# Outputs of a pair and scores of the next in one visit of TensorE, with another plan of steps and another order at the seam

## The reference

```python
batch, n_heads, seq, head_dim = (4, 8, 768, 48)      # d_model 384
for t in range(S):                                     # per batch b and head h
    state = alpha[:, :, t, :, None] * state + einsum('bhd,bhe->bhde', k[:, :, t], v[:, :, t])
    y[:, :, t] = einsum('bhd,bhde->bhe', q[:, :, t], state)
x = y.transpose(0, 2, 1, 3).reshape(B * S, H * D)      # 3072 tokens x 384
g = relu(x @ moe_w_in) ** 2;  x = g @ moe_w_out        # d_ff 2048
h = x @ moe2_w_in;            out = silu(h) @ moe2_w_out
```

## Time and profile before

| | us |
|---|---|
| median of 3 runs | 881.25 (881.04 to 883.57) |
| the profiled execution, its own time | 879.24 |
| its span | 877.6 |
| PE busy with products | 862.9 (98% of the span) |
| DVE busy | 542.7 (62%) |
| ACT busy | 436.4 (50%) |
| granted clock of PE | full in the whole span |

### The profile page before, as it was taken

How to read it: one execution, slowest core, us unless ns; L and a number is a source line. 1 busy time by engine, 2 the same in 40 slices (tenths; PEclk the granted TensorE clock), 3 DMA queues, 4 the chain that set the end, 5 groups by cost and what they waited for, 6 DMA issues and landing times.

```text
span 877.6 us, 17615 instructions
## 1 busy us (share of the span) xinstructions
PE 862.9 (98%) x6834; PEld 707.4 (81%) x6834; DVE 542.7 (62%) x1072; ACT 436.4 (50%) x770; POOL 104.5 (12%) x127
## 2 busy tenths in 40 slices
PE   6999989999999999999999999999999999999998
PEld 6777768788878788788888788888888888888898
DVE  7788876777767667664344556556855445766620
ACT  5765544455446445544666644445534436554510
POOL 3453300000000000000344003003030003000000
PEclk9999999999999999999999999999999999999999
DMA  8985424333333332300412362000130000110010
GB/s 171 239 227 124 99 66 120 74 75 103 71 82 87 101 79 67 103 19 15 147 49 66 61 116 72 0 1 1 44 102 0 1 1 1 36 37 1 1 48 28
DMA packets 134203, 60.03 MB, mean 68 GB/s; under 512 B 81824, under 2 KB 129312, under 8 KB 134112
## 3 DMA queue, kind: packets, MB, share of 16 engines
q1 hardware_dynamic: 130800, 58.14, 26.9%
q10 hardware_dynamic: 3312, 0.69, 0.4%
HBM read 45.02 MB, written 9.44 MB: 62 GB/s over the span
## 4 chain that ended last, share of the span: by engine, by line
PE 93%; DVE 4%; issue 1%; ACT 1%; DMA 0%; DVEq 0%; ACTq 0%
PE z_ps L1146 21%; PE h_ps L1132 21%; PE h_ps L1175 20%; PE z_ps L1211 11%; PE jobs L1211 7%; PE jobs L1231 3%; PE jobs L1007 1%; PE jobs L1040 1%; PE jobs L1109 1%; DVE decay L1703 1%; PE jobs L1018 1%; PE jobs L1117 1%; PE h_ps L1231 1%; DVE decay L1688 1%; PE z_ps L1078 0%
## 5 line engine op out<-in xcount | busy, mean ns | idle before, releaser
L1429 ACT ACTIVATE g<-h_ps 128x512 f32<-128x512 f32 x96 | 57.4, 597 | 177.6 <-PE h_ps L1132 175.5
L1523 ACT ACTIVATE sum<-sum 128x512 f32<-128x512 f32 x96 | 60.5, 630 | 139.0 <-DVE sum L1871 115.1
L1810 DVE TENSOR_TENSOR g_lo<-g,g_hi 128x512 fp32r<-128x512 f32 x96 | 67.5, 704 | 85.4 <-ACT g L1435 85.4
L1871 DVE TENSOR_TENSOR sum<-h_ps,sum 128x512 f32<-128x512 f32 x120 | 82.8, 691 | 54.2 <-PE h_ps L1175 51.6
L1132 PE MATMUL h_ps<-x_hi,win_hi 128*128 128x512 f32 x288 | 115.0, 399 | 1.2 <-ACT g L1429 0.8
L1146 PE MATMUL z_ps<-g_hi,wout_hi 128*128 128x512 f32 x282 | 114.4, 406 | 0.0
L1132 PE MATMUL h_ps<-x_hi,win_lo 128*128 128x512 f32 x288 | 112.4, 390 | 0.0
L1132 PE MATMUL h_ps<-x_lo,win_hi 128*128 128x512 f32 x288 | 112.2, 389 | 0.0
L1146 PE MATMUL z_ps<-g_hi,wout_lo 128*128 128x512 f32 x282 | 110.2, 391 | 0.0
L1146 PE MATMUL z_ps<-g_lo,wout_hi 128*128 128x512 f32 x282 | 110.1, 390 | 0.0
L1175 PE MATMUL h_ps<-s_hi,t_hi 128*128 128x512 f32 x264 | 103.3, 391 | 0.8 <-DVE sum L1871 0.8
(11 more groups left out here) (169 smaller groups left out, 1544.1 us busy)
## 6 DMA issues: line engine op xcount, KB each, us to landing
z_scratch<-z_sb SPq DMA_DIRECT2D x18, 256.0 KB, 2.6
pre<-z_scratch SPq DMA_DIRECT2D x18, 256.0 KB, 3.8
v_sb<-in_v SPq DMA_DIRECT2D x44, 96.0 KB, 2.6
out_x<-z_stage SPq DMA_DIRECT2D x80, 48.0 KB, 1.7
nat_a<-in_alpha SPq DMA_DIRECT2D x40, 88.0 KB, 2.3
nat_k<-in_k SPq DMA_DIRECT2D x40, 88.0 KB, 2.4
nat_q<-in_q SPq DMA_DIRECT2D x40, 88.0 KB, 2.3
nat_a<-in_alpha SPq DMA_DIRECT2D x40, 80.0 KB, 2.7
```

Source lines behind the costliest of these rows:

```text
L1429: nc.scalar.activation(g[f % 2][:], h_ps[f % 2][:], ACT.Relu).then_inc(act_made, 1)
L1523: nc.scalar.activation(at[:], at[:], ACT.Silu).then_inc(silu_made, 1)
L1810: nc.vector.tensor_tensor(low, g[f % 2][:], high.bitcast(F32), ALU.subtract).then_inc(g_lo_made, 1)
L1871: nc.vector.tensor_tensor(to[:], h_ps[(PRODUCTS * n + r) % 2][:], other[:], ALU.add).then_inc(summed, 1)
```

## The change

Three things change.

1. *One visit.* For pairs n = 8 and later, Y(n) stands in the step of S(n + 1), and ahead of it on PE, so that both are made in one visit between the first and the second product. The output part from the state no longer goes to job_ps[2] but to the bank of h that the step before used (`later_y(n)`), and so S no longer waits for the addition of y. In its place, Y waits for the relu that read that bank and for the addition of the pair before, and the first product of the next step, which writes that bank again, waits for the addition of this y. ACT's copy of y and DVE's addition, which spanned both banks in one instruction, become two each. DVE does the additions right behind the masks of the scores.
2. *Another plan of steps.* Pairs 8 to 11 have their S in steps 16, 18, 21, 24 (before 16, 18, 22, 26), their A in 13, 16, 19, 22 (before 13, 16, 19, 23) and KQ in 14, 17, 20, 23 (before 14, 17, 21, 25). Pairs 12 and later have S in 4 n - 20 in place of 4 n - 18, A in 4 n - 23 in place of 4 n - 21, KQ in 4 n - 21 in place of 4 n - 19. Y(n) stays in 4 n - 16 from pair 11 on.
3. *The seam.* In group 0 ACT copies the last z banks behind the bank of P5 instead of ahead of it; in the first 8 groups DVE adds the bank of P3 ahead of v_lo instead of behind it.

```diff
@@ stage_step
-    if n == 2 * PAIRS:
-        return {"A": 13, "KQ": 14, "S": 16, "I": 16, "Y": 17}[kind]
-    return {"A": -20 if n == 2 * PAIRS + 1 else -21, "KQ": -19, "S": -18, "I": -18, "Y": -16}[kind] + 4 * n
+    if kind == "Y":
+        return stage_step("S", n + 1)
+    if n < 3 * PAIRS:
+        return {"A": (13, 16, 19, 22), "KQ": (14, 17, 20, 23), "S": (16, 18, 21, 24), "I": (16, 18, 21, 24)}[kind][n - 2 * PAIRS]
+    return {"A": -23, "KQ": -21, "S": -20, "I": -20}[kind] + 4 * n
@@ beside
-    return sorted(jobs, key=lambda j: ("S", "I", "A", "Y", "KQ").index(j[0]))
+    return sorted(jobs, key=lambda j: ("Y", "S", "I", "A", "KQ").index(j[0]))
+def beside_scores(n):
+    return n >= 2 * PAIRS
@@ build
-        first_y, middle_y, later_y = z_ps[1], z_ps[0], (job_ps[2], job_ps[0])
+        first_y, middle_y = z_ps[1], z_ps[0]
+        def later_y(n):
+            return (h_ps[(stage_step("Y", n) - 1) % 2][:] if beside_scores(n) else job_ps[2], job_ps[0])
@@ PE, s_stage
-                if n > PAIRS:
+                if n > PAIRS and not beside_scores(n - 1):
                     wait(pe, y_copied, y_count(n))
@@ PE, y_halves
+                if beside_scores(n):
+                    wait(pe, y_copied, y_count(n))
+                    wait(pe, act_made, stage_step("Y", n))
@@ PE, loop over the steps, ahead of first_product
+                for kind, n in beside(F - 1):
+                    if kind == "Y" and beside_scores(n):
+                        pe.wait_ge(y_copied, y_count(n + 1))
@@ ACT, y_copy
+                if beside_scores(n):
+                    to = y_sb[n % 2][:].rearrange("p (c k t) -> p k c t", c=BATCH, k=2)
+                    for k in (0, 1):
+                        last = nc.scalar.activation(to[:, k], later_y(n)[k][0:ROWS, UT // 2:].rearrange("p (c t) -> p c t", c=BATCH),
+                                                    ACT.Copy)
+                    last.then_inc(within_copied, 1)
+                    return
@@ ACT, group n of the second layer
                 tile_step(n, C11)
-                if n == 0:
-                    copy_z(UNITS - 1, UNITS - 1, UNITS - 1)
...
                 spread_second(n)
...
                 if q == 0:
                     for f in v_group(j):
                         v_split(f)
+                if n == 0:
+                    copy_z(UNITS - 1, UNITS - 1, UNITS - 1)
                 tile_step(n, C12)
@@ DVE, y_stage
+                if beside_scores(n):
+                    for k in (0, 1):
+                        to = y_sb[n % 2][:, k * UT // 2:(k + 1) * UT // 2]
+                        last = nc.vector.tensor_tensor(to, later_y(n)[k][0:ROWS, 0:UT // 2], to, ALU.add)
+                    last.then_inc(y_copied, 1)
+                    return
@@ DVE, loop over the steps
                 for kind, n in jobs_here:
                     if kind == "S":
                         s_stage(n)
+                for kind, n in jobs_here:
+                    if kind == "Y" and beside_scores(n):
+                        y_stage(n)
+                for kind, n in jobs_here:
                     if kind == "KQ":
...
-                    if kind == "Y" and n != 2 * PAIRS - 1:
+                    if kind == "Y" and n != 2 * PAIRS - 1 and not beside_scores(n):
                         y_stage(n)
@@ DVE, group n of the second layer
+                dve.wait_ge(summed, PRODUCTS * n + U4_AT)
+                from_bank(n, P3, s_b[2], s_b[2])
                 if q == 0:
                     for f in v_group(j):
                         low_v(f)
-                dve.wait_ge(summed, PRODUCTS * n + U4_AT)
-                from_bank(n, P3, s_b[2], s_b[2])
```

More of the change, by code:

```diff
@@ L1103, in to @@
                     rows = slice(0, 64) if b < 2 else head_rows(1)
-                    return later_y[bank][rows, place * HALF:(place + 1) * HALF], 64 if b < 2 else HD
+                    return later_y(n)[bank][rows, place * HALF:(place + 1) * HALF], 64 if b < 2 else HD
                 for half in (0, 1):
```

## The result

| | before | changed |
|---|---|---|
| median, us | 881.79 (878.98 to 884.40, 22 runs) | 884.46 (881.57 to 889.18, 22 runs) |
| the profiled execution, its own time | 879.24 | 882.96 |
| its span | 877.6 | 881.2 |

The ratio of changed to before is 1.0033, with a 95% interval of 1.0024 to 1.0043: slower by 0.3%.

A forecast was written before the change was run, and what follows sets the result against it. PE, busy 862.9 of 877.6 us, was taken as the bound. Terms -3.4 - 2.5 + 1.5 + 4.5 + 5.4 - 0.9 = +4.6 took 879.24 to 883.8, a median of 886.0 us; range 878.5 to 891.

The forecast's parts named there:

- Visits: On PE, Y(8) to Y(22) join S(9) to S(23): 15 visits fewer at 0.23 us each, -3.4 us.
- Old and new wait of S(9): In step 18, S(9) stops waiting for y's addition, -2.5 us, but waits for q instead, +1.5 us.
- S(10) and S(11): With pairs 10 and 11 three steps apart, both scores wait 2.3 us for q, behind DVE's queue: +4.5 us.
- Rival 1: The new waits do not come, DVE's chain to q being 2.3 us shorter; median 876, chance 0.15.
- Unit edges: At pairs 13, 17, 21 the split of x enters the chain to q: 1.8 us three times, +5.4 us.
- y's addition at no cost: The two y additions end 1.0 us before the next first product starts, so they cost nothing.
- Seam: In the first Strassen group, the new order of copies and additions starts P4 at 502.9 instead of 503.76: -0.9 us.
- rival 4: PE's clock falls to its lower level for one step after each of five new waits: +20 us, median 906, chance 0.02.
- From the profiled execution to the median: The median of timed runs was taken to stand 2.0 us above the profiled execution: 883.8 became 886.0.

The follow-up runs named there:

- e6: e3 with outputs made ahead of the last three of nine large first products and scores behind them, so visits are separate again; 879.98 us, ratio 0.9982 to before.
- e1: The changed kernel with A(10) and A(11) one step earlier (18 and 21); 878.59 us, ratio 0.9956 to the kernel before.
- e2: The changed kernel with A(13), A(17), A(21) one step earlier (28, 44, 60); 879.83 us, ratio 0.9977 to the kernel before.
- e10: e3 with DVE's additions of y about 0.9 us later, ahead of the rest of the I work; 872.34 us, ratio 0.9890 to the kernel before.
- e7: e3 with DVE adding y behind its work for the state instead of right behind the masks; 911.75 us, ratio 1.0336 to the kernel before.
- e4: The kernel before with only the new order at the seam; 880.92 us, ratio 0.9985 to the kernel before.
- e9: e3 with four extra transposes of k on DVE for six pairs, to make their scores wait; 885.40 us, ratio 1.0038 to the kernel before.
- e8: e3 with five extra transposes of k on DVE for six pairs, to make their scores wait; 897.68 us, ratio 1.0187 to the kernel before.
- e3: The changed kernel with A one step earlier for every pair from 10 on; 871.90 us, ratio 0.9889 to the kernel before.
- e5: e3 with S(9) to S(11) in steps 19, 22, 25, pairs 8 to 11 evenly spaced; 871.78 us, ratio 0.9885 to the kernel before.

## Why the prediction was right, and where its terms were off

- **Visits**, forecast -3.4, measured -5.4. The mechanism was right, the size off. The term counted only the 0.23 of a single visit and took the 1.08 of the small work as fixed. In a joined visit the outputs take 0.97, 0.11 less; e6 gave both parts back. This stood within the bounds of 0 to -6.9.
- **Old and new wait of S(9)**, forecast -2.5 and +1.5, measured the same. Here and for S(10) and S(11) two parts were off and cancelled, which is luck: S starts 0.10 after q is ready (122.60 and 122.70), where 0.26 was taken over from the wait for y, and PE comes 0.11 earlier, because Y is shorter.
- **S(10) and S(11)**, forecast +4.5, measured +4.6, and e1 shows the cause: with A ahead of the g_lo that waits for ACT, both are gone. Rival 1 of the prediction named this very difference (in the earlier pairs, three steps apart as well, A stands in the score step itself), without drawing the remedy from it.
- **Unit edges**, forecast +5.4, measured +5.1, and e2 shows the cause. The 1.8 of each came as 1.57 at S, and 0.14 ahead of the new unit's first product, which needs the split x and which I hadn't named. Whether x_hi or x_lo held it there wasn't tried.
- **y's addition at no cost**, cover forecast 1.0, measured 1.2 (161.83 + 0.42 = 162.25 against 163.42). e10 shortened it to 0.3 at no cost, and e7 used it up and paid up to 2.0 a step. The two additions take 0.75 together, as forecast, against 0.68 for the one.
- **Seam**, forecast -0.9, measured -1.1 in the whole and 0.66 in the gap before P4 alone. e4's ratio, 1.3 us of 882.0, agrees, but its interval reaches from 0.2 to 2.6.
- **The clock** (rival 4) was put at 0.02 and at +20 us. The step that failed is the reading of the earlier trace rows: one stretch at full clock was taken to show that such waits are free. It was also the wrong stretch, for it ends at 124.00 and S(9) starts at 124.21: it holds the wait and what stands ahead of it. The same view of the kernel before for the time behind the wait shows the full clock as well, so in that one execution the statement happened to be true:

```profile
124.00:126.00 2.00, 1.79 (x67) 1.68 (x68) 0.42 (x2) 0.00 (x0) 0.00 (x0) 1.00 0.13 39
126.00:128.00 2.00, 2.00 (x38) 1.41 (x38) 1.20 (x4) 0.49 (x1) 0.00 (x0) 1.00 0.31 81
```

But such waits are not free: about 1.5 us is paid behind some of them, in some executions. A fall of the kind seen in step 21 takes the mean clock of an execution to 0.998. Only two of the changed kernel's 22 executions, and four of the 23 of the kernel before that ran beside e1 to e4, have a mean clock of 0.999 or 1.000. A mean of 0.999 goes without such a fall in the profiles of e1 and e6: there the clock is low only at the very end, when PE is done and the last transfer lands.

- **From the profiled execution to the median** I added 2.0, as a mere offset. At least two things stand behind it, about 1.5 us each. One is that same clock: the kernel before spans 877.4 in the executions with a clock of 1.000, close to the profiled 877.6, and 878.7 or more in the others. The other is the last transfer of the output, which landed 1.2 to 1.8 us later in half of the twelve profiles. Spans at the same mean clock still differ by 2 us and more (the changed kernel's two at 1.000: 879.8 and 881.8), and what makes these up in the unprofiled executions isn't recorded.

The total was forecast as +4.6 and came as +3.7 in the profiled executions: -2.0 for the visits, -0.2 for the seam, -0.3 for the edges and +0.1 for the dense pairs against +1.5 for the clock. That the sum came so near is in part luck, since the visits and the clock were off by 2.0 and 1.5 in opposite directions.

The Trainium skill (TensorE: Matmul & The Clock Gate, "The HAM clock gate") has the array at 1.2 GHz once it has been idle, and says that the moment of a change varies from run to run. The traces agree with the first in kind: the lower level came only behind idle stretches. The page warns of idle gaps longer than any of these waits of 1.49 to 2.65 us; there it and the measurement differ, and the measurement decides. On the second, what varies here is whether a fall comes at all: of waits of 1.41 and 1.49 us in one execution (e9), one brought the lower clock and the other not.

## What to carry to other kernels

When a change joins work or takes a visit away, follow what each engine's queue does with the job that feeds it: here DVE's scans stood one g_lo too late, and moving one job by one step turned 1.0033 into 0.9889. Read a wait marked "issue" beside the timeline of the engine that should feed it. And count a wait of 1.5 us or more of the matrix engine as costing perhaps 1.5 us beyond itself: half of those seen here did, and a single profile may not show it.

## What was not expected of the hardware

- Behind waits of 1.5 to 2.7 us in the middle of dense work the granted clock went to 1.2 GHz in some cases, for about 3 us: large products 0.43 apart instead of 0.227, 1.5 to 1.6 us lost. It happened in the profiles of the changed kernel, of e2, e4, e7, e8 and e9, within 1.9 us of the wait's end.
- 64 small products take 0.97 us with small ones behind them and 1.08 with a large one behind them, whatever bank they write.
- The last output transfer of 96 KB landed after 1.7 us in the profiles of the kernel before, the changed kernel, e2, e3, e5 and e10, and after 2.9 to 3.5 us in those of e1, e4, e6, e7, e8 and e9, with the same work ahead of it. The cause is open.
